# First tile's rows gathered straight into the output buffer, second tile's directly behind, and GpSimd's expert work in one loop

## The reference

```python
# 1. delta-rule attention, 4 x 8 heads, 768 steps, head size 48
y[:, :, t] = einsum('bhd,bhde->bhe', q[:, :, t], state)
state = state + bt * einsum('bhd,bhe->bhde', kt, vt - einsum('bhde,bhd->bhe', state, kt))
# 2. MLP on 3072 tokens of width 384, hidden 2048
h = x @ w_in;  x = (h * sigmoid(h)) @ w_out
# 3. mixture of experts: 8 experts, hidden 1024, one expert per token, some tokens skip it
do_compute = (x @ w_skip) > 0
e_idx = argmax(x @ w_gate);  gate_w = softmax(x @ w_gate)[e_idx]
for e in range(8):
    y[e_idx == e] = gate_w * (relu(x[e_idx == e] @ w1[e]) @ w2[e])
out = x;  out[do_compute] = x[do_compute] + y
```

## Time and profile before

| | us |
|---|---|
| three runs | 831.6, 833.06 (median), 836.32 |
| the profiled execution, its own time | 830.03 |
| its span, first to last instruction | 828.4 |
| PE busy | 781.3 (94%) |
| DVE busy | 570.7 (69%) |
| ACT busy | 360.3 (43%) |
| POOL busy | 133.8 (16%) |
| expert part, first up matmul to last output | 659.6 to 817.2 |
| from the last output to the last instruction | 11.2 |

### The profile page before, as it was taken

One profiled execution on the slowest core, in us unless ns is written; L12 is line 12 of the kernel. 1 busy time (PEld: TensorE's weight loads), 2 busy tenths in 40 slices (PEclk: granted clock), 3 DMA queues, 4 the chain that ended last, 5 costly groups with the idle time before them and its releaser, 6 DMA issues.

```text
span 828.4 us, 28842 instructions
## 1 busy us (share of the span) xinstructions
PE 781.3 (94%) x12083; PEld 713.8 (86%) x12083; DVE 570.7 (69%) x1503; ACT 360.3 (43%) x1024; POOL 133.8 (16%) x313
## 2 busy tenths in 40 slices
PE   5988899999999999999999999999999969999993
PEld 3557798999999988999999999999999869999993
DVE  6989888778776876878678776544334647767751
ACT  3734433434345343544434344443444445555531
POOL 1000000010020100101010010101012145555561
PEclk9999999999999999999999999999999989999997
DMA  8772021121302212112211202110134454656610
GB/s 276 221 235 84 23 85 41 67 91 54 104 22 66 73 66 91 48 65 66 77 62 41 91 22 74 57 47 21 41 114 142 142 180 163 198 181 187 191 32 14
DMA packets 48096, 79.84 MB, mean 96 GB/s; under 512 B 5840, under 2 KB 35498, under 8 KB 47968
## 3 DMA queue, kind: packets, MB, share of 16 engines
q1 hardware_dynamic: 44544, 73.07, 27.3%
q0 software_dynamic: 3424, 4.93, 1.9%
HBM read 67.05 MB, written 13.19 MB: 97 GB/s over the span
## 4 chain that ended last, share of the span: by engine, by line
issue 75%; POOL 12%; DMA 6%; PE 3%; DVE 1%; POOLq 1%; ACT 0%; SPq 0%
DMA id_table<-token,slot 5%; POOL idle L691 4%; POOL kq_t L746 3%; POOL id_table L736 2%; PE psum L996 2%; POOL out L806 1%; POOL kq_t L787 1%; POOL ids_all L742 1%; POOL ids_all L797 1%; PE psum L852 1%; DMA id_table<-x_sb 1%; DMA kd<-kq 0%; POOLq L527 0%; PE psum L997 0%; POOLq L768 0%
## 5 line engine op out<-in xcount | busy, mean ns | idle before, releaser
L1030 PE MATMUL psum<-xt_hi,w_hi 128*128 128x256 f32 x768 | 225.4, 293 | 2.0 <-DVE xt_lo L1571 1.0
L1031 PE MATMUL psum<-xt_lo,w_hi 128*128 128x256 f32 x768 | 217.1, 283 | 0.0
L1032 PE MATMUL psum<-xt_hi,w_lo 128*128 128x256 f32 x768 | 216.9, 282 | 0.0
L1206 ACT ACTIVATE h_raw<-psum 128x256 f32<-128x256 f32 x192 | 73.7, 384 | 318.3 <-PE psum L1032 316.7
L1461 DVE TENSOR_TENSOR h_lo<-h_raw,h_hi 128x256 fp32r<-128x256 f32 x192 | 81.3, 423 | 156.2 <-ACT h_hi L1207 155.3
L1030 PEld LDWEIGHTS psum<-xt_hi,w_hi 128*128 128x128 f32 x768 | 144.8, 189 | 9.3 <-issue 2.2
L1032 PEld LDWEIGHTS psum<-xt_hi,w_lo 128*128 128x128 f32 x768 | 145.8, 190 | 0.0
L1031 PEld LDWEIGHTS psum<-xt_lo,w_hi 128*128 128x128 f32 x768 | 145.3, 189 | 0.0
L1054 PE MATMUL psum<-w_hi,h_hi 128*128 128x394 f32 x384 | 138.5, 361 | 0.8 <-DVE h_lo L1461 0.8
L691 POOL TENSOR_TENSOR idle<-half 1x1 f32<-1x1 f32 x141 | 38.7, 288 | 610.8 <-PE psum L928 465.6
L1055 PE MATMUL psum<-w_lo,h_hi 128*128 128x394 f32 x384 | 131.2, 342 | 0.0
(11 more groups left out here) (187 smaller groups left out, 1106.5 us busy)
## 6 DMA issues: line engine op xcount, KB each, us to landing
kq_t<-kq SPq DMA_DIRECT2D x24, 512.0 KB, 3.4
bp<-moe_w SPq DMA_DIRECT2D x24, 512.0 KB, 4.0
kv_t<-kv SPq DMA_DIRECT2D x24, 384.0 KB, 3.1
bp<-moe_w SPq DMA_DIRECT2D x24, 384.0 KB, 4.6
kd<-kq SPq DMA_DIRECT2D x20, 256.0 KB, 3.3
x_table<-x_sb SPq DMA_DIRECT2D x13, 392.0 KB, 2.9
out<-x_sb SPq DMA_DIRECT2D x12, 384.0 KB, 3.2
bp<-moe_w_in SPq DMA_DIRECT2D x6, 512.0 KB, 5.9
```

The costliest lines, as they stand in the source:

```text
L1030: m(out, hi, x_hi, start=first, stop=False)
L1031: m(out, hi, x_lo, start=False, stop=False)
L1032: return m(out, lo, x_hi, start=False, stop=last)
L1206: a_.activation(h_raw[i % 2][:, :], up_ps[i % 2][:, 0:G2], ACT.Silu)
```

## The change

Three edits, all in the expert part.

1. Ahead of the loop, tile 0's rows are gathered straight into `xg` (own semaphore `xg_first`), and its copy goes. The load of tile 1's id list (own semaphore `next_in`) is issued ahead of that gather, and tile 1's gather into `xg_in` directly behind it. Tile 2's id list is loaded ahead of the wait for `xg_first`.
2. GpSimd has one loop over tiles 1 to 7, with the number of tiles read once. One pass t is: wait for y of tile t-1; copy; gather tile t+1; scatter tile t-1; pass the ids on; load the id list of tile t+2. The last tile's scatter follows behind the loop.
3. VectorE's L1609 waits for `rows_moved` (the scatters' own semaphore) where it waited for `ids_copied`. Counts of `xg_gathered` are lower by one gather, on TensorE too.

```diff
-            load_ids(0, ids_next, first_in)
+            load_ids(0, ids, first_in)
+            pool.wait_ge(starts_ready, 1)
+            load_ids_of(1, ids_next, next_in)
             pool.wait_ge(table_stored, 16 * NP)
             pool.wait_ge(out_stored, 16 * NP)
+            hold(first_in, 32)
+            gather_rows(ids, xg, xg_first)
             hold(xgt_ps[1], 1)
-            hold(first_in, 32).then_inc(ids_free, 1)
-            gather_rows(ids_next, xg_gathered)
-            pool.wait_ge(starts_ready, 1)
-            load_ids_of(1)
-            hold(xg_gathered, 32)
-
-            def one(e, i, more, first, last_t):
-                with pool.Fori(first, last_t) as t:
-                    hold(y_ready, t + 1)
-                    hold(xg_gathered, t * 32 + 32)
-                    for a in range(2):
-                        last = g.tensor_copy(xg[a], xg_in[a])
-                    last.then_inc(xg_copied, 1)
-                    hold(xg_copied, t + 1)
-                    hold(xgt_ps[1], t + 1)
-                    hold(ids_loaded, t * 16 + 16)
-                    gather_rows(ids_in, xg_gathered)
-                    hold(rows_moved, t * 32 + 32)
-                    hold(ids_free, t + 1)
-                    g.tensor_copy(ids, ids_next).then_inc(ids_copied, 1)
-                    hold(xg_gathered, t * 32 + 64)
-                    hold(ids_copied, t + 1)
-                    g.tensor_copy(ids_next, ids_in).then_inc(ids_free, 1)
-                    hold(ids_free, t + 2)
-                    load_ids_of(t + 2)
-                    hold(y_ready, t + 2)
-                    for a in range(2):
-                        g.indirect_dma_start(out=out[:, :], ...).then_inc(rows_moved, 16)
-
-            experts(pool, one)
-            last_tile = pool.value_load(ends[0:1, E:E + 1], min_val=1, max_val=MAXT)
+            hold(next_in, 16)
+            gather_rows(ids_next, xg_in, xg_gathered)
+            load_ids_of(2, ids_in, ids_loaded)
+            hold(xg_first, 32).then_inc(xg_copied, 1)
+
+            pool.wait_ge(plan_ready, 1)
+            last_tile = pool.value_load(ends[0:1, E:E + 1], min_val=E, max_val=MAXT)
+            with pool.Fori(1, last_tile) as t:
+                hold(y_ready, t + 1)
+                hold(xg_gathered, t * 32)
+                for a in range(2):
+                    last = g.tensor_copy(xg[a], xg_in[a])
+                last.then_inc(xg_copied, 1)
+                hold(xg_copied, t + 1)
+                hold(xgt_ps[1], t + 1)
+                hold(ids_loaded, t * 16)
+                gather_rows(ids_in, xg_in, xg_gathered)
+                scatter_rows()
+                hold(rows_moved, t * 32 + 32)
+                g.tensor_copy(ids, ids_next).then_inc(ids_copied, 1)
+                hold(xg_gathered, t * 32 + 32)
+                hold(ids_copied, t)
+                g.tensor_copy(ids_next, ids_in).then_inc(ids_free, 1)
+                hold(ids_free, t)
+                load_ids_of(t + 2, ids_in, ids_loaded)
+
+            hold(y_ready, last_tile + 1)
+            scatter_rows()
             hold(rows_moved, last_tile * 32 + 32)
-            hold(ids_loaded, last_tile * 16 + 16)
+            hold(ids_loaded, last_tile * 16)
+            hold(xg_gathered, last_tile * 32)
...
             def transposes(t, a):
-                pe.wait_ge(xg_gathered, t * 32 + 32)
+                pe.wait_ge(xg_gathered, t * 32)
...
-                    dve.wait_ge(ids_copied, t + 1)
+                    dve.wait_ge(rows_moved, t * 32 + 32)
```

More of the change, by code:

```diff
@@ L275, in program @@
         rows_moved, ids_free = sem("rows_moved"), sem("ids_free")
+        xg_first, next_in = sem("xg_first"), sem("next_in")
         place_step = sem("place_step")
@@ L742, in load_ids, with gather_rows @@
                 g.dma_start(to, id_table[bass.ds(at, G2), :].rearrange("(p a) n -> p (a n)", a=2)).then_inc(loaded, 16)
-            def gather_rows(which, gathered):
+            def gather_rows(which, to, gathered):
                 for a in range(2):
-                    g.indirect_dma_start(out=xg_in[a], out_offset=None, in_=x_table[:, :],
+                    g.indirect_dma_start(out=to[a], out_offset=None, in_=x_table[:, :],
                                          in_offset=bass.IndirectOffsetOnAxis(ap=which[:, a:a + 1], axis=0),
@@ L760, in first @@
                     pool.wait_ge(rows_there, 16)
-                    gather_rows(ids_in, rows_moved)
+                    gather_rows(ids_in, xg_in, rows_moved)
             schedule(steps(turn=turn, place=place, first=first))
@@ L765, in _, with load_ids_of, scatter_rows @@
             hold(id_stored, 32 * NP)
-            def load_ids_of(t):
-                load_ids(pool.value_load(starts[0:1, bass.ds(t, 1)], min_val=0, max_val=E * N - G2), ids_in, ids_loaded)
-            load_ids(0, ids_next, first_in)
+            def load_ids_of(t, to, loaded):
+                load_ids(pool.value_load(starts[0:1, bass.ds(t, 1)], min_val=0, max_val=E * N - G2), to, loaded)
+            def scatter_rows():
+                for a in range(2):
+                    g.indirect_dma_start(out=out[:, :], out_offset=bass.IndirectOffsetOnAxis(ap=ids[:, a:a + 1], axis=0),
+                                         in_=y_sb[a], in_offset=None, bounds_check=N - 1,
+                                         oob_is_err=False).then_inc(rows_moved, 16)
@@ L778, in _ @@
-            hold(xg_gathered, 32)
-            def one(e, i, more, first, last_t):
-                with pool.Fori(first, last_t) as t:
-                    hold(y_ready, t + 1)
-                    hold(xg_gathered, t * 32 + 32)
-                    for a in range(2):
-                        last = g.tensor_copy(xg[a], xg_in[a])
-                    last.then_inc(xg_copied, 1)
-                    hold(xg_copied, t + 1)
-                    hold(xgt_ps[1], t + 1)
-                    hold(ids_loaded, t * 16 + 16)
-                    gather_rows(ids_in, xg_gathered)
-                    hold(rows_moved, t * 32 + 32)
-                    hold(ids_free, t + 1)
-                    g.tensor_copy(ids, ids_next).then_inc(ids_copied, 1)
-                    hold(xg_gathered, t * 32 + 64)
-                    hold(ids_copied, t + 1)
-                    g.tensor_copy(ids_next, ids_in).then_inc(ids_free, 1)
-                    hold(ids_free, t + 2)
-                    load_ids_of(t + 2)
-                    hold(y_ready, t + 2)
-                    for a in range(2):
-                        g.indirect_dma_start(out=out[:, :], out_offset=bass.IndirectOffsetOnAxis(ap=ids[:, a:a + 1], axis=0),
-                                             in_=y_sb[a], in_offset=None, bounds_check=N - 1,
-                                             oob_is_err=False).then_inc(rows_moved, 16)
```

## The result

| | before | after |
|---|---|---|
| median of the runs with the result | 833.51 us (4 runs) | 822.31 us (818.78 to 824.12, 4 runs) |
| ratio | | 0.9858, 95% interval 0.9813 to 0.9903 |
| the same kernel in a later series (16 and 6 runs) | 834.13 | 820.18, ratio 0.983, 0.9803 to 0.9858 |
| profiled execution, its own time | 830.03 | 824.12 |

What follows compares the result with a forecast made beforehand. TensorE, busy 94%, was taken as the bound, so gains were its waits: 8.57 + 4.32 = 12.9, less 0.3, 0.2 and 0.15, a gain of 12.2 us; forecast 820.5 us, range 816.5 to 825.5.

Steps and rivals of the forecast that it cites:

- Second gather directly behind the first: Tile 0: issuing tile 1's gather earlier cuts a late-gather cost of 8.57 us to a 0.3 wait; gain 8.3.
- Gather ahead of the scatter: Tiles 1 to 7: gathers land before TensorE needs them; 4.32 us of waits go, less 0.2 for a bad landing.
- such a wait would not lower the clock: Tile 0: a wait of up to 2.4 us at TensorE's transposes would leave the granted clock at 1.00.
- rival A: Tile 0: the second gather lands late and TensorE waits 2.4 us; gain 10.1, time 822.9; chance 0.12.
- Scatter behind the gather: Loop: the scatter is issued 3 to 5 us later but lands before VectorE's next output needs it; cost 0.
- First gather into `xg`: Tile 0: removes one GpSimd copy (0.96 us) and its holds; counted at nothing.
- One loop: GpSimd: register loads between experts' loops go; worth 0 to 0.5 us of GpSimd time, off the path.
- The end: After the last output: one hold more ahead of the final instruction; cost 0.15 us.
- Sum: Expert part (E, first up matmul of tile 0 to last instruction): all terms together, a gain of 12.2 us.
- rival B: Tiles 1 to 7: the steady waits stay, tiles keep about 18.4 us; gain 8.1, time 824.9; chance 0.11.
- its signs: Trace marks for right, including tile 0's output at about 679.9, last output at 804.8, no tile 0 wait above 0.5.
- C: Loop: VectorE's output waits for the later scatter; if it lands at 19.5 us, time 840.5; chance 0.03.

Runs made afterwards that it cites:

- kept_busy: The kernel before the change, with 56 unused matmuls on TensorE ahead of the transposes, filling tile 0's wait; 828.98 us, ratio 0.9944.
- again: The changed kernel unaltered, run once more; ratio 0.983 to the kernel before.
- old_wait: The changed kernel with VectorE's output waiting for `ids_copied` again; tiles 1 to 7 took 124.82 us, against 124.71 in the changed kernel.
- order_only: The kernel before with the one loop and the gather ahead of the scatter, but the old start in tile 0; ratio 0.9889 to the kernel before.
- prologue_only: The changed kernel with the scatter again ahead of copy and gather in the loop, the new start kept; 824.97 us, ratio 0.9888 to the kernel before.
- late_scatter_20: The changed kernel with 20 one-element GpSimd multiplies between gather and scatter in each pass; tiles 1 to 7 took 135.81 us, against 124.71.

## Why the prediction was right, point by point

- *Second gather directly behind the first*: forecast 8.3, measured 8.5 (28.58 to 20.10). The mechanism holds: the wait is gone, and kept_busy shows that 1.7 of it were the clock. The steps of the chain were less well told, and their errors cancel, which is luck. Counted from the first up matmul, the first gather was to keep its start at 4.4 us and started at 5.2, as a register load and an id load stand ahead of it now; its issue took 2.5 us for 3.2, so it ended at 7.7 for 7.6. The gap to the second was 1.6 us for 0.5 to 0.9, since two holds took 1.41. The second's issue took 1.03 + 0.30 + 0.99, the lower bound, where I had added 0.6 for a meeting with a split. So it ended at 11.56, where 11.45 was forecast. The landing then took at most 4.3 us in this trace, and 5.1 to 5.2 in again and old_wait. The wait that I put at 0.3 was 0 to 0.92.
- *Gather ahead of the scatter*: forecast 4.1, measured 4.35; order_only has it alone, with the same 124.71. Against other executions of the old order it is worth 2.4 to 7.5. The 4.32 was one draw of a quantity that varies, and I took it for a constant; that the forecast hit it is luck. The step "such a wait would not lower the clock", read from one tile that kept 1.00, does not hold in general: prologue_only's tile 4 lost 1.5 us to the clock behind a wait of 1.85. So a wait of 2.4, as in rival A, could have cost more than its length.
- *Scatter behind the gather*: forecast to land 9 to 12.4 us behind the output, measured 12.3 in the first pass and 13.4 in the fifth, beyond the far end. Two errors cancel in part: it was issued from 4.9 us behind the output, where 5 to 7.6 was forecast, but took 6.1 us from the issue of its second half to landing, where I had 2.5 to 3.4. Behind the same kind of gather, but with the weight loads over, it took 4.3 (781.62 to 785.93). So some of the rise goes with the loads and some is there without them; how much the gather ahead of it adds was not tested by itself. The cost is 0, as forecast. But I had named 4 us of slack on the output and 1 to 6 on the id list, and not that of GpSimd's own pass, which late_scatter_20 shows to be the one that decides. It was 2.6 us in most passes, but 1.06 in the fifth here and 0.48 in the fifth of old_wait (scatter landed 14.1 behind the output). That margin was thin, and the prediction did not see it.
- *First gather into `xg`, the direct wait*: cost 0, as forecast; old_wait shows it for the wait. The first of the two was tested only together with the rest of the new start. *One loop*: put at nothing, which holds where the second gather no longer waits for the copy; with the old start it is part of a gain of 3 us. The split between it and the quicker landing there is argued from one trace, not shown.
- *The end*: forecast +0.15, measured +0.1.
- Sum: E forecast to fall by 12.2, measured 12.7. The total came 1.8 us above the forecast in the first four runs and 0.3 below it in the next six. The profiled execution was forecast at 817.8 and took 824.12: its lead was 6.6 longer, which the prediction had no term for. A run like that lay in the range only because the range reached to rival B's 824.9. For the same reason two of its signs missed by their clock time (tile 0's output at 686.28 for 679.9, the last output at 810.99 for 804.8) and hold once counted from the first up matmul (20.10 for 20.35, 144.81 for 145.25).
- Rivals: A happened in small (0.92 and 0.87 us in two profiles, 0.8 to 0.9 on tile 0; above the 0.5 that was the sign for right, below the 2 that was the sign for wrong). B did not: no tile above 17.84. C did not, but it is real and nearer than I priced it: 4.9 us on the scatter gave 11 us back.

## What to carry to other kernels

When an in-order queue carries both a transfer that the bottleneck waits for and one that nobody needs soon, issue the first ahead of the second, and count the whole pass of that queue: its idle time at the end of a pass is the slack, and a delay beyond it is paid again in each pass. Take it from the tightest pass, not from the first. A stall on TensorE can cost more than its length: here 6.78 us cost 1.7 more, 3.75 cost 1.45 more, and of two stalls of 1.8 one cost 1.5 more and one nothing. Measure the stretch from its end to the next known event against an undisturbed one. And compare kernels by the stretch that the change touches, if the rest of the program varies by more than the gain.

## What the runs showed of the hardware

- A GpSimd copy (0.5 us a half) that starts just ahead of a VectorE subtraction of two SBUF tensors held it up (1.93 for 1.21 us); an indirect DMA's issue that started 0.05 us ahead of the same subtraction did not (1.23, and 1.06 for the issue). In the other order the subtraction held up the indirect DMA (1.92 for 1.07).
- 20 one-element multiplies on GpSimd took 4.9 us beside VectorE's splits, 0.25 each, and 2.94 in late_scatter_20's last pass, without them, 0.15 each.
- In order_only, behind 3.75 us without a matmul, the granted clock was 0.56, near its lower level, and tile 0 lost 1.45 us beside them (25.30 - 20.10 - 3.75). Its stretches, the wait and what came behind it:

```profile
675.00:678.75 3.75, 0.00 (x1) 0.00 (x1) 1.20 (x3) 0.10 (x1) 1.36 (x2) 0.97 0.96 334
678.75:682.40 3.65, 3.65 (x15) 3.65 (x16) 1.11 (x2) 1.18 (x3) 0.00 (x0) 0.56 0.12 43
```
